# Attention scores from two query tiles stacked in the 128 rows, with the low part of k made after the transpose

## The chip, the cores and the metric

The kernel runs on one core of a Trainium2 chip. The metric is the device time of one execution in microseconds; the times below are medians of several executions of the same program. A profile is one further execution, recorded by the hardware profiler. Six actors matter: TensorE (PE, with its weight loads as PEld), VectorE (DVE), ScalarE (ACT), GpSimd (Pool), and the DMA queues, here issued by SyncE (SP). Each engine works through its own list of instructions in order, and semaphores tie the lists together.

## The reference

Three layers follow each other. The change touches the first alone: attention with normalised queries and keys, 4 x 12 = 48 heads of 448 tokens and 64 columns, in float32.

```python
def rmsnorm(x, g):
    rms = np.sqrt(np.mean(x * x, axis=-1, keepdims=True) + 1e-06)
    return x / rms * g
q_n, k_n = (rmsnorm(q, g_q), rmsnorm(k, g_k))
scores = (1.0 / np.sqrt(64)) * np.matmul(q_n, k_n.transpose(0, 1, 3, 2))
scores = scores - np.max(scores, axis=-1, keepdims=True)
attn = np.exp(scores)
attn = attn / (np.sum(attn, axis=-1, keepdims=True) + 1e-09)
out = np.matmul(attn, v)
```

Behind it come a mixture of 8 experts (each token goes to one) and a feed-forward layer of 768 x 2048. Both are left as they are.

## The kernel before

The kernel runs four stages in a row: `attention`, `routing`, `experts`, `feed_forward`. Attention loops over N = 48 heads. A head has T = 4 tiles of R = 112 tokens; D is 64. float32r matmuls take a float32 operand rounded to a shorter mantissa, so an operand is split into a high and a low part (`_hi`, `_lo`), whose products are summed in PSUM.

One head n goes through these steps; `m` is the loop variable, and each engine's loop (lines 197, 278, 363 and 458) sets its order by hand, with pieces of several heads in one iteration:

- ACT squares q and k (L311). DVE sums each row's 64 squares (L394). Pool turns the sums into 1/rms (L159, L161).
- Pool multiplies k by it (k_n, L177), again with a rounded output (the high half of `k_hl`, L183), and subtracts for the low half (L187). `k_hl` thus holds high and low side by side, 128 columns. Pool also writes the normalised q twice side by side into `q_n` (L193).
- PE transposes k's four tiles into the one bank `ps_tr` (L229); ACT copies them to `kT` (L329): rows 0 to 63 hold the high part, rows 64 to 127 the low part. Then PE transposes q's four tiles into the same bank (L236, it has to wait for `kT`); ACT rounds them to `qT_hi` and multiplies by the gain (L337); DVE makes `qT_lo` (L411).
- Scores: for each tile t one bank of `ps_s`, by two matmuls of 128 rows and 448 columns, `qT_hi` and `qT_lo` against `kT` (L221, L222).
- DVE takes the row maximum (L401), ACT the exponential with its row sum (L346), PE transposes it into `ps_pt` (L244, two banks in turn), ACT rounds (L355), DVE subtracts (L407). These four steps run once per tile.
- Values: eight matmuls of 112 rows and 448 columns into `ps_ux` (L258, L259), in two parts of four. ACT copies the result (`copy_u`, L317), PE multiplies by `mix` into the same bank (`outputs`, L266, eight instructions in the trace), and DVE scales it into `x_tok` (L421). v is split by ACT (L323, it waits for the values of the head before) and Pool (L147).

SP's queue loads q and k of head n once Pool has used those of head n-2, then v, then stores an older head. In one iteration, PE runs scores of tiles 2 and 3 (head m), the transposes of k (m+1), p of tile 0 (m), the first half of the values (m-1), the transposes of q (m+1), the second half of the values, p of tiles 1 and 2, scores of tiles 0 and 1 (m+1), p of tile 3 (m), and the outputs (m-1).

## Time and profile before

| what | value |
|---|---|
| median of 3 runs | 1293.96 us (1291.87 to 1294.43) |
| profiled execution, its own time | 1296.19 us |
| its span, first to last instruction | 1294.5 us |
| mean granted TensorE clock over the span | 0.973 |

The span lies 1.69 us under the profiled execution's own time, and that time 2.23 us over the median. Attention fills the span's first 350 us: the first exponential starts at 18.08 us, the last head's first one at 339.01 us. Rows of a timeline give start, duration, engine, line, operation and shapes. An engine's next instruction may start before the last has ended; so the cost of an instruction on its engine is the distance from its start to the next start, and its duration counts for whoever waits for the result. "Idle" in brackets is the engine's wait before the row, and who ended it.

### The profile page before, as it was taken

The page shows a single profiled execution, that of the slowest core. Times are in us where ns is not written, and L with a number is a line of the kernel's source. Part 1 is how long each engine was busy: PE and PEld are TensorE (multiplying, and loading weights), DVE is VectorE, ACT ScalarE, POOL GpSimd, SP SyncE. Part 2 cuts the span into 40 slices and gives each one's busy share as a digit, 9 for nine tenths or more (in the row PEclk, how much of TensorE's full clock was granted, in tenths as well). Part 3 has the DMA queues.
Part 4 walks back from the last instruction along what each step waited for, and adds up shares of the span by engine and source line. Part 5 has one row for each costly group of instructions (what it writes and reads, how often), then busy time and mean ns, then how long its engine had stood idle before and what let it go on. Part 6 is the DMA issues. An engine that isn't in the chain of part 4 may idle for free. (4 is left out here: it accounts for less than half of the span.)

```text
span 1294.5 us, 21003 instructions
## 1 busy us (share of the span) xinstructions
PE 1226.4 (95%) x6890; PEld 1097.1 (85%) x6890; DVE 894.2 (69%) x1257; ACT 757.6 (59%) x1434; POOL 553.3 (43%) x581
## 2 busy tenths in 40 slices
PE   5999999999748999999999995999999999999998
PEld 4888888888637988998899884999999999999997
DVE  4999999999757999999999973554432245552222
ACT  4999999999748777877787754222331122221111
POOL 6888888888335777667766740000000000000000
PEclk8999999999959999999999996999999999999999
DMA  1234333322103643664364014112232322211122
GB/s 50 75 103 116 97 105 93 83 67 72 29 28 120 244 142 128 244 244 147 124 242 147 38 49 122 49 49 62 74 92 62 91 65 74 70 44 49 56 86 73
DMA packets 99977, 126.42 MB, mean 98 GB/s; under 512 B 28568, under 2 KB 81048, under 8 KB 99872
## 3 DMA queue, kind: packets, MB, share of 16 engines
q1 hardware_dynamic: 92416, 103.07, 26.0%
q0 software_dynamic: 3360, 16.52, 3.5%
q10 hardware_dynamic: 4096, 5.51, 1.2%
q8 instruction: 57, 0.93, 0.3%
q14 instruction: 48, 0.39, 0.1%
HBM read 193.88 MB, written 19.27 MB: 165 GB/s over the span
## 5 line engine op out<-in xcount | busy, mean ns | idle before, releaser
L1010 ACT CAST w_hi<-w_raw 128x768 fp32r<-128x768 f32 (+1 forms) x294 | 249.7, 931 | 14.5 <-DMA w_raw<-moe_w_in 13.4
L1080 DVE TENSOR_TENSOR w_lo<-w_raw,w_hi 128x1024 fp32r<-128x1024 f32 x84 | 186.9, 2261 | 9.7 <-POOL w_lo L899 7.0
L1490 DVE TENSOR_TENSOR out_lo<-out_raw,out_hi 128x384 fp32r<-128x384 f32 x64 | 35.7, 558 | 169.5 <-ACT out_hi L1399 169.5
L1281 PE MATMUL ps_acc<-yT_hi,in_hi 128*128 128x448 f32 x384 | 142.9, 372 | 2.1 <-DVE yT_lo L1476 2.1
L899 POOL TENSOR_TENSOR w_lo<-w_raw,w_hi 128x1024 fp32r<-128x1024 f32 x42 | 105.8, 2520 | 91.3 <-ACT w_hi L1010 91.0
L1311 PE MATMUL ps_acc<-gT_hi,out_hi 128*128 128x448 f32 x384 | 142.6, 371 | 0.0
L1393 ACT ACTIVATE small_h<-ps_acc 128x448 f32<-128x448 f32 x64 | 34.9, 545 | 183.4 <-PE ps_acc L1283 183.4
L1282 PE MATMUL ps_acc<-yT_hi,in_lo 128*128 128x448 f32 x384 | 141.9, 370 | 0.0
L1283 PE MATMUL ps_acc<-yT_lo,in_hi 128*128 128x448 f32 x384 | 141.9, 369 | 0.0
L1313 PE MATMUL ps_acc<-gT_lo,out_hi 128*128 128x448 f32 x384 | 140.5, 366 | 0.0
L1312 PE MATMUL ps_acc<-gT_hi,out_lo 128*128 128x448 f32 x384 | 140.4, 366 | 0.0
L1399 ACT CAST out_hi<-out_raw 128x384 fp32r<-128x384 f32 x64 | 32.8, 513 | 179.9 <-PE ps_acc L1313 179.6
L1089 DVE TENSOR_TENSOR w_lo<-w_raw,w_hi 128x768 fp32r<-128x768 f32 x126 | 135.1, 1137 | 0.0
L407 DVE TENSOR_TENSOR pT_lo<-ps_pt,pT_hi 112x448 fp32r<-112x448 f32 x192 | 115.1, 620 | 27.6 <-ACT pT_hi L355 27.5
L346 ACT ACTIVATE probs<-ps_s,neg_max 112x448 f32<-112x448 f32 x192 | 122.7, 644 | 3.6 <-DVE neg_max L401 3.6
L1498 DVE TENSOR_TENSOR g_sb<-ps_acc,small_h 128x448 f32<-128x448 f32 x64 | 40.0, 625 | 116.3 <-ACT small_h L1393 116.3
L983 PE MATMUL ps_y<-w_hi,hT_hi 128*128 128x384 f32 x336 | 116.8, 348 | 1.5 <-issue 1.3
L893 POOL TENSOR_TENSOR w_lo<-w_raw,w_hi 128x768 fp32r<-128x768 f32 x42 | 105.7, 2518 | 22.9 <-ACT w_hi L1010 21.4
L401 DVE TENSOR_REDUCE neg_max<-ps_s 112x1 f32<-112x448 f32 x192 | 113.3, 610 | 2.0 <-PE ps_s L222 1.8
L984 PE MATMUL ps_y<-w_lo,hT_hi 128*128 128x384 f32 x336 | 113.5, 338 | 0.0
L985 PE MATMUL ps_y<-w_hi,hT_lo 128*128 128x384 f32 x336 | 113.5, 338 | 0.0
L953 PE MATMUL ps_h<-w_hi,xT_hi 128*128 128x512 f32 x252 | 101.3, 402 | 4.8 <-DVE w_lo L1080 2.9
(182 smaller groups left out, 2999.7 us busy)
## 6 DMA issues: line engine op xcount, KB each, us to landing
w_raw<-moe_w_in SPq DMA_DIRECT2D x84, 1536.0 KB
in_raw<-moe_w_in_in SPq DMA_DIRECT2D x32, 384.0 KB, 3.3
out_raw<-moe_w_out_in SPq DMA_DIRECT2D x64, 192.0 KB, 2.4
qk_raw<-q_in SPq DMA_DIRECT2D x48, 112.0 KB, 2.1
qk_raw<-k_in SPq DMA_DIRECT2D x48, 112.0 KB, 2.2
v_raw<-v_in SPq DMA_DIRECT2D x48, 112.0 KB, 2.0
x_rows<-x_tok SPq DMA_DIRECT2D x48, 112.0 KB, 2.5
out_rows<-o_sb ACTq DMA_DIRECT2D x26, 168.0 KB, 2.4
```

What stands on the lines that cost most here:

```text
L346: act.activation(probs[:, t, :], ps_s[0:R, t, 0:S], ACT.Exp, bias=neg_max[u][:, t:t + 1], accum_out=sums[u][:, t:t + 1]).then_inc(s_exp, 1)
L407: dve.tensor_tensor(pT_lo[u][:, :, cols], src, pT_hi[u][:, :, cols].bitcast(F32), ALU.subtract).then_inc(s_plo, 1)
L983: pe.matmul(out, hT_hi[u][:, c, :], w2_hi[:, c, cols], start=c == 0, stop=False)
L1010: act.copy(out[:, c, :], raw[:, c, :]).then_inc(s_hi, 1)
L1080: dve.tensor_tensor(w1_lo[:, c, :], w1_raw[:, c, :], w1_hi[:, c, :].bitcast(F32), ALU.subtract).then_inc(s_w1lo, 1)
L1089: dve.tensor_tensor(w2_lo[:, c, :], w2_raw[:, c, :], w2_hi[:, c, :].bitcast(F32), ALU.subtract).then_inc(s_w2lo, 1)
L1281: pe.matmul(h, in_hi[u][:, c, :], yT_hi[:, c, cols], start=c == 0, stop=False)
L1282: pe.matmul(h, in_lo[u][:, c, :], yT_hi[:, c, cols], start=False, stop=False)
L1283: last = pe.matmul(h, in_hi[u][:, c, :], yT_lo[:, c, cols], start=False, stop=c == C - 1)
L1311: pe.matmul(acc, out_hi[u][:, lhs], hi, start=first, stop=False)
L1312: pe.matmul(acc, out_lo[u][:, lhs], hi, start=False, stop=False)
L1313: last = pe.matmul(acc, out_hi[u][:, lhs], lo, start=False, stop=final)
```

## The change

Scores no longer contract 128 rows of high and low k. k is transposed unsplit, written twice side by side by Pool (`k_nn`), so that both halves of the 128 rows of the transposed bank hold the same 64 rows. ACT rounds this to `kT_hi`, and DVE subtracts to make `kT_lo` (new `split_k`, L411 of the kernel after; its instructions are 128x448). q is written once; one transpose takes two tiles of q side by side, so tile 2g lands in rows 0 to 63 and tile 2g+1 in rows 64 to 127, and `qT_hi`, `qT_lo` have 224 columns. For each pair g there are six matmuls of 64 rows and 448 columns, three into each of two banks, in turn from the upper and the lower rows. DVE's row sums of squares get their input halved by a new addition on Pool (`fold_squares`).

Orders change too: ACT's `square` stands at the end of the iteration, one head further ahead; PE's two halves of the values stand together ahead of the transposes of q; DVE's `split_k` stands behind the row maximum of tile 3.

```diff
@@ pool @@
+            def fold_squares(n, u):
+                pool.wait_ge(s_sq, n + 1)
+                if n > 1:
+                    pool.wait_ge(s_ss, n - 1)
+                pool.tensor_tensor(folded[u][:, :, :], squares[u][:, :, 0:D // 2], squares[u][:, :, D // 2:D], ALU.add).then_inc(s_fold, 1)
+
             def norm_k(n, u):
                 pool.wait_ge(s_r, n + 1)
-                if n > 0:
-                    pool.wait_ge(s_khl, n)
-                pool.tensor_tensor(k_n[:, :, :], qk_raw[u][:, 1, :, :], factors(u, 1), ALU.mult).then_inc(s_kn, 1)
-
-            def norm_k_hi(n, u):
-                pool.wait_ge(s_kn, n + 1)
                 if n > 1:
                     pool.wait_ge(s_trk, n - 1)
-                pool.tensor_tensor(k_hl[u][:, :, 0, :], qk_raw[u][:, 1, :, :], factors(u, 1), ALU.mult).then_inc(s_khi, 1)
-
-            def split_k(n, u):
-                pool.wait_ge(s_khi, n + 1)
-                pool.tensor_tensor(k_hl[u][:, :, 1, :], k_n[:, :, :], k_hl[u][:, :, 0, :].bitcast(F32), ALU.subtract).then_inc(s_khl, 1)
+                for a in range(2):
+                    last = pool.tensor_tensor(k_nn[u][:, :, a, :], qk_raw[u][:, 1, :, :], factors(u, 1), ALU.mult)
+                last.then_inc(s_kn, 1)
 
             def norm_q(n, u):
                 if n > 1:
                     pool.wait_ge(s_trq, n - 1)
-                for a in range(2):
-                    last = pool.tensor_tensor(q_n[u][:, :, a, :], qk_raw[u][:, 0, :, :], factors(u, 0), ALU.mult)
-                last.then_inc(s_qn, 1)
+                pool.tensor_tensor(q_n[u][:, :, :], qk_raw[u][:, 0, :, :], factors(u, 0), ALU.mult).then_inc(s_qn, 1)
...
@@ tensor @@
-            def scores(n, u, t):
+            def scores(n, u, g):
+
                 if n > 0:
-                    pe.wait_ge(s_exp, (n - 1) * T + t + 1)
-                if t == 0:
+                    pe.wait_ge(s_exp, (n - 1) * T + 2 * g + 2)
+                if g == 0:
                     pe.wait_ge(s_qlo, n + 1)
-                cols = slice(t * R, (t + 1) * R)
-                pe.matmul(ps_s[0:R, t, 0:S], qT_hi[u][:, cols], kT[u][:, :], start=True, stop=False)
-                pe.matmul(ps_s[0:R, t, 0:S], qT_lo[u][:, cols], kT[u][:, :], start=False, stop=True).then_inc(s_s, 1)
+                cols = slice(g * R, (g + 1) * R)
+                for i, (qT, kT) in enumerate(((qT_hi, kT_hi), (qT_hi, kT_lo), (qT_lo, kT_hi))):
+                    for half in range(2):
+                        rows = slice(half * D, (half + 1) * D)
+                        last = pe.matmul(ps_s[0:R, 2 * g + half, 0:S], qT[u][rows, cols], kT[u][rows, :], start=i == 0, stop=i == 2)
+                last.then_inc(s_s, 2)
...
             def transpose_q(n, u):
                 pe.wait_ge(s_qn, n + 1)
-                pe.wait_ge(s_kT, n + 1)
-                for t in range(T):
-                    last = pe.transpose(ps_tr[:, t * R:(t + 1) * R], q_n[u][:, t, :, :].rearrange("p a d -> p (a d)"), ident[0:R, 0:R])
+                pe.wait_ge(s_klo, n + 1)
+                for g in range(T // 2):
+                    two = q_n[u][:, 2 * g:2 * g + 2, :].rearrange("p a d -> p (a d)")
+                    last = pe.transpose(ps_tr[:, g * R:(g + 1) * R], two, ident[0:R, 0:R])
                 last.then_inc(s_trq, 1)
...
@@ scalar @@
-                act.copy(kT[u][:, :], ps_tr[:, 0:S]).then_inc(s_kT, 1)
+                act.copy(kT_hi[u][:, :], ps_tr[:, 0:S]).then_inc(s_khi, 1)
...
-                act.activation(qT_hi[u][:, :], ps_tr[:, 0:S], ACT.Copy, scale=gain[:, 0:1]).then_inc(s_qhi, 1)
+                act.activation(qT_hi[u][:, :], ps_tr[:, 0:S // 2], ACT.Copy, scale=gain[:, 0:1]).then_inc(s_qhi, 1)
...
@@ vector @@
-                dve.tensor_reduce(sumsq[u][:, :], squares[u][:, :, :], AX.X, ALU.add).then_inc(s_ss, 1)
+                dve.tensor_reduce(sumsq[u][:, :], folded[u][:, :, :], AX.X, ALU.add).then_inc(s_ss, 1)
...
+            def split_k(n, u):
+                dve.wait_ge(s_khi, n + 1)
+                dve.tensor_tensor(kT_lo[u][:, :], ps_tr[:, 0:S], kT_hi[u][:, :].bitcast(F32), ALU.subtract).then_inc(s_klo, 1)
```

**PE, middle of an iteration.** The rows stand from p of tile 0 to the end of the values; L244/L246 transpose p, L258 to L261 are the values, L236/L238 the transposes of q. Before:

```order
L244 MATMUL ps_pt<-ident,probs 112x112 x3
L258 MATMUL ps_ux<-pT_hi,v_hl 128x448 [waits s_vhl,s_plo,s_xc]
L259 MATMUL ps_ux<-pT_lo,v_hl 128x448
L258 MATMUL ps_ux<-pT_hi,v_hl 128x448
L259 MATMUL ps_ux<-pT_lo,v_hl 128x448
L236 MATMUL ps_tr<-ident,q_n 128x112 [waits s_kT,s_qn]
L236 MATMUL ps_tr<-ident,q_n 128x112 x3
L258 MATMUL ps_ux<-pT_hi,v_hl 128x448
L259 MATMUL ps_ux<-pT_lo,v_hl 128x448
L258 MATMUL ps_ux<-pT_hi,v_hl 128x448
L259 MATMUL ps_ux<-pT_lo,v_hl 128x448
```

After:

```order
L246 MATMUL ps_pt<-ident,probs 112x112 x3
L260 MATMUL ps_ux<-pT_hi,v_hl 128x448 [waits s_vhl,s_plo,s_xc]
L261 MATMUL ps_ux<-pT_lo,v_hl 128x448
L260 MATMUL ps_ux<-pT_hi,v_hl 128x448
L261 MATMUL ps_ux<-pT_lo,v_hl 128x448
L260 MATMUL ps_ux<-pT_hi,v_hl 128x448
L261 MATMUL ps_ux<-pT_lo,v_hl 128x448
L260 MATMUL ps_ux<-pT_hi,v_hl 128x448
L261 MATMUL ps_ux<-pT_lo,v_hl 128x448
L238 MATMUL ps_tr<-ident,q_n 128x112 [waits s_klo,s_qn]
L238 MATMUL ps_tr<-ident,q_n 128x112
```

The transposes of q have moved behind all eight matmuls of the values; they are two, not four, and wait for DVE's `s_klo` in place of ACT's `s_kT`.

**ACT, one iteration** from the exponential of tile 2 to the next copy of transposed k. L346/L345 are the exponentials, L355/L354 the rounding of p, L311/L310 the squares. Before:

```order
L346 ACTIVATE probs,sums<-ps_s,neg_max 112x448 [waits s_pt,s_max]
L355 CAST pT_hi<-ps_pt 112x4x112 [waits s_u,s_pt]
L337 ACTIVATE qT_hi<-ps_tr,gain 128x448 [waits s_s,s_trq]
L323 CAST v_hl<-v_raw 112x4x64 [waits s_u,s_v_in0]
L355 CAST pT_hi<-ps_pt 112x4x112 [waits s_pt]
L346 ACTIVATE probs,sums<-ps_s,neg_max 112x448 [waits s_pt,s_max]
L317 COPY u_sb<-ps_ux 128x448 [waits s_x,s_u]
L355 CAST pT_hi<-ps_pt 112x4x112 [waits s_pt] x2
L346 ACTIVATE probs,sums<-ps_s,neg_max 112x448 [waits s_se,s_pt,s_max]
L346 ACTIVATE probs,sums<-ps_s,neg_max 112x448 [waits s_pt,s_max]
L311 ACTIVATE squares<-qk_raw 112x512 [waits s_ss,s_qk_in0]
L329 CAST kT<-ps_tr 128x448 [waits s_s,s_trk]
```

After:

```order
L345 ACTIVATE probs,sums<-ps_s,neg_max 112x448 [waits s_pt,s_max]
L354 CAST pT_hi<-ps_pt 112x4x112 [waits s_u,s_pt]
L336 ACTIVATE qT_hi<-ps_tr,gain 128x224 [waits s_s,s_trq]
L322 CAST v_hl<-v_raw 112x4x64 [waits s_u,s_v_in0]
L354 CAST pT_hi<-ps_pt 112x4x112 [waits s_pt]
L310 ACTIVATE squares<-qk_raw 112x512 [waits s_fold,s_qk_in0]
L345 ACTIVATE probs,sums<-ps_s,neg_max 112x448 [waits s_pt,s_max]
L316 COPY u_sb<-ps_ux 128x448 [waits s_x,s_u]
L354 CAST pT_hi<-ps_pt 112x4x112 [waits s_pt] x2
L345 ACTIVATE probs,sums<-ps_s,neg_max 112x448 [waits s_se,s_pt,s_max]
L345 ACTIVATE probs,sums<-ps_s,neg_max 112x448 [waits s_pt,s_max]
L328 CAST kT_hi<-ps_tr 128x448 [waits s_s,s_trk]
```

The squares have moved from behind the exponential of tile 1 to a place between the copy of q and the exponential of tile 3.

**DVE, from the store of x to the split of q.** L401 is the row maximum, L407 the low part of p. Before:

```order
L421 TENSOR_TENSOR x_tok<-ps_ux,inv_sums 112x4x72 [waits s_rs,s_x]
L401 TENSOR_REDUCE neg_max<-ps_s 112x1 [waits s_s]
L394 TENSOR_REDUCE sumsq<-squares 112x8 [waits s_ms,s_sq]
L416 RECIPROCAL inv_sums<-sums_eps 112x4 [waits s_se]
L401 TENSOR_REDUCE neg_max<-ps_s 112x1 [waits s_s]
L407 TENSOR_TENSOR pT_lo<-ps_pt,pT_hi 112x4x112 [waits s_phi]
L411 SCALAR_TENSOR_TENSOR qT_lo<-ps_tr,gain,qT_hi 128x448 [waits s_qhi]
```

After:

```order
L425 TENSOR_TENSOR x_tok<-ps_ux,inv_sums 112x4x72 [waits s_rs,s_x]
L401 TENSOR_REDUCE neg_max<-ps_s 112x1 [waits s_s]
L394 TENSOR_REDUCE sumsq<-folded 112x8 [waits s_ms,s_fold]
L420 RECIPROCAL inv_sums<-sums_eps 112x4 [waits s_se]
L401 TENSOR_REDUCE neg_max<-ps_s 112x1 [waits s_s]
L411 TENSOR_TENSOR kT_lo<-ps_tr,kT_hi 128x448 [waits s_khi]
L407 TENSOR_TENSOR pT_lo<-ps_pt,pT_hi 112x4x112 [waits s_phi]
L415 SCALAR_TENSOR_TENSOR qT_lo<-ps_tr,gain,qT_hi 128x224 [waits s_qhi]
```

The new subtraction stands behind the row maximum of tile 3, ahead of the low part of p.

## Rows read from the trace of the kernel before

**Rows 1.** The page: span, then busy time of each engine.

```profile
span 1294.5 us, 21003 instructions
PE 1226.4 (95%) x6890; PEld 1097.1 (85%) x6890; DVE 894.2 (69%) x1257; ACT 757.6 (59%) x1434; POOL 553.3 (43%) x581
```

**Rows 2.** Busy time by stretch of attention; columns in the first row.

```profile
core 0: us, PE busy (x) PEld busy (x) DVE busy (x) ACT busy (x) POOL busy (x), PEclk, DMA share, GB/s
20.00:30.00 10.00, 8.22 (x44) 6.52 (x44) 8.03 (x14) 5.64 (x16) 5.92 (x10) 0.70 0.18 51
...
128.00:196.00 68.00, 67.73 (x485) 58.46 (x484) 61.87 (x122) 66.38 (x172) 57.78 (x92) 1.00 0.37 98
```

**Rows 3.** Line of the squares, 60 to 340 us: count, first and last start.

```profile
L311 ACT ACTIVATE squares<-qk_raw x40: 633/635/637, 64.2 to 326.8; 112x512 f32<-112x512 f32 x40
```

**Rows 4.** Timeline of PE, one head: start, us, engine, line, operation.

```profile
156.18 0.57 PE L244 MATMUL ps_pt<-ident,probs 112*112 112x112 f32 x4
156.59 0.92 PE L266 MATMUL ps_ux<-mix,u_sb 128*112 128x72 f32 x8
157.30 0.44 PE L221 MATMUL ps_s<-kT,qT_hi 128*112 128x448 f32 x1
...
158.20 0.55 PE L229 MATMUL ps_tr<-ident,k_hl 112*128 112x112 f32 x4
...
158.90 0.45 PE L258 MATMUL ps_ux<-pT_hi,v_hl 112*128 112x448 f32 x1
...
159.80 0.55 PE L236 MATMUL ps_tr<-ident,q_n 112*128 112x112 f32 x4
...
160.60 0.36 PE L258 MATMUL ps_ux<-pT_hi,v_hl 112*128 112x448 f32 x1
160.80 0.36 PE L259 MATMUL ps_ux<-pT_lo,v_hl 112*128 112x448 f32 x1
161.01 0.93 PE L244 MATMUL ps_pt<-ident,probs 112*112 112x112 f32 x8
```

**Rows 5.** Timeline of ACT, the same head.

```profile
155.27 0.64 ACT L346 ACTIVATE probs<-ps_s,neg_max 112x448 f32<-112x448 f32 x1
...
155.89 0.53 ACT L317 COPY u_sb<-ps_ux 128x448 f32<-128x448 f32 x1
160.41 0.68 ACT L337 ACTIVATE qT_hi<-ps_tr,gain 128x448 fp32r<-128x448 f32 x1
161.26 0.41 ACT L323 CAST v_hl<-v_raw 112x256 fp32r<-112x256 f32 x1 [0.17 <-PE ps_ux L259]
161.59 0.53 ACT L355 CAST pT_hi<-ps_pt 112x448 fp32r<-112x448 f32 x1
162.02 0.64 ACT L346 ACTIVATE probs<-ps_s,neg_max 112x448 f32<-112x448 f32 x1
```

**Rows 6.** Timeline of ACT in the last full head, which has no squares.

```profile
332.28 0.64 ACT L346 ACTIVATE probs<-ps_s,neg_max 112x448 f32<-112x448 f32 x1
...
333.84 0.53 ACT L329 CAST kT<-ps_tr 128x448 fp32r<-128x448 f32 x1 [0.21 <-PE ps_tr L229]
...
339.01 0.64 ACT L346 ACTIVATE probs<-ps_s,neg_max 112x448 f32<-112x448 f32 x1
```

**Rows 7.** Timeline of DVE, the head of rows 4.

```profile
157.01 1.15 DVE L407 TENSOR_TENSOR pT_lo<-ps_pt,pT_hi 112x448 fp32r<-112x448 f32 x2
...
158.44 0.61 DVE L401 TENSOR_REDUCE neg_max<-ps_s 112x1 f32<-112x448 f32 x1
159.11 0.69 DVE L394 TENSOR_REDUCE sumsq<-squares 112x8 f32<-112x512 f32 x1
...
159.80 0.60 DVE L401 TENSOR_REDUCE neg_max<-ps_s 112x1 f32<-112x448 f32 x1
```

**Rows 8.** SP's queue in the same head, then line L99's time from issue to landing.

```profile
159.37 0.43 SPq L99 DMA_DIRECT2D qk_raw<-k_in  x1
...
DMA to landing us min/median/max: 1.9/2.1/3.1
```

More of the change, by code:

```diff
@@ L46, in attention @@
         eps_d = sb("eps_d", [R, 2 * T])
-        q_n = [sb(f"q_n{u}", [R, T, 2, D]) for u in range(2)]
-        k_n = sb("k_n", [R, T, D])
-        k_hl = [sb(f"k_hl{u}", [R, T, 2, D], F32R) for u in range(2)]
+        folded = [sb(f"folded{u}", [R, 2 * T, D // 2]) for u in range(2)]
+        q_n = [sb(f"q_n{u}", [R, T, D]) for u in range(2)]
+        k_nn = [sb(f"k_nn{u}", [R, T, 2, D]) for u in range(2)]
         v_hl = [sb(f"v_hl{u}", [R, T, 2, D], F32R) for u in range(2)]
-        kT = [sb(f"kT{u}", [P, S], F32R) for u in range(2)]
-        qT_hi = [sb(f"qT_hi{u}", [P, S], F32R) for u in range(2)]
-        qT_lo = [sb(f"qT_lo{u}", [P, S], F32R) for u in range(2)]
+        kT_hi = [sb(f"kT_hi{u}", [P, S], F32R) for u in range(2)]
+        kT_lo = [sb(f"kT_lo{u}", [P, S], F32R) for u in range(2)]
+        qT_hi = [sb(f"qT_hi{u}", [P, S // 2], F32R) for u in range(2)]
+        qT_lo = [sb(f"qT_lo{u}", [P, S // 2], F32R) for u in range(2)]
         neg_max = [sb(f"neg_max{u}", [R, T]) for u in range(2)]
@@ L80, in attention @@
         s_v_in = [sem(f"s_v_in{u}") for u in range(2)]
[L81 to L83 removed]
+        s_half, s_sq, s_fold, s_ss, s_ms, s_r = (sem(x) for x in ("s_half", "s_sq", "s_fold", "s_ss", "s_ms", "s_r"))
+        s_qn, s_kn, s_vhi, s_vhl = (sem(x) for x in ("s_qn", "s_kn", "s_vhi", "s_vhl"))
+        s_trk, s_khi, s_klo, s_trq, s_qhi, s_qlo = (sem(x) for x in ("s_trk", "s_khi", "s_klo", "s_trq", "s_qhi", "s_qlo"))
         s_s, s_max, s_exp, s_pt, s_phi, s_plo = (sem(x) for x in ("s_s", "s_max", "s_exp", "s_pt", "s_phi", "s_plo"))
@@ L191, in norm_q @@
                     pool.wait_ge(s_trq, n - 1)
-                for a in range(2):
-                    last = pool.tensor_tensor(q_n[u][:, :, a, :], qk_raw[u][:, 0, :, :], factors(u, 0), ALU.mult)
-                last.then_inc(s_qn, 1)
+                pool.tensor_tensor(q_n[u][:, :, :], qk_raw[u][:, 0, :, :], factors(u, 0), ALU.mult).then_inc(s_qn, 1)
             pool.wait_ge(s_half, 3)
             for m in range(-2, N):
+                if m + 2 < N:
+                    fold_squares(m + 2, (m + 2) % 2)
                 if 0 <= m + 1 < N:
-                    split_k(m + 1, (m + 1) % 2)
                     norm_q(m + 1, (m + 1) % 2)
@@ L228, in transpose_k @@
                 for t in range(T):
-                    last = pe.transpose(ps_tr[:, t * R:(t + 1) * R], k_hl[u][:, t, :, :].bitcast(F32).rearrange("p a d -> p (a d)"), ident[0:R, 0:R])
+                    last = pe.transpose(ps_tr[:, t * R:(t + 1) * R], k_nn[u][:, t, :, :].rearrange("p a d -> p (a d)"), ident[0:R, 0:R])
                 last.then_inc(s_trk, 1)
@@ L279, in _ @@
                 if 0 <= m < N:
-                    scores(m, m % 2, 2)
-                    scores(m, m % 2, 3)
+                    scores(m, m % 2, 1)
                 if m + 1 < N:
@@ L287, in _ @@
                     values(m - 1, (m - 1) % 2, 0)
+                    values(m - 1, (m - 1) % 2, 1)
                 if m + 1 < N:
                     transpose_q(m + 1, (m + 1) % 2)
-                if m - 1 >= 0:
-                    values(m - 1, (m - 1) % 2, 1)
                 if 0 <= m < N:
@@ L296, in _ @@
                     scores(m + 1, (m + 1) % 2, 0)
-                    scores(m + 1, (m + 1) % 2, 1)
                 if 0 <= m < N:
@@ L386, in _ @@
                     split_hi(m, m % 2, 1)
+                if m + 3 < N:
+                    square(m + 3, (m + 3) % 2)
+                    square_emb(m + 3, (m + 3) % 2)
         @block.vector
@@ L472, in _ @@
                     row_max(m, m % 2, 3)
+                if 0 <= m + 1 < N:
+                    split_k(m + 1, (m + 1) % 2)
+                if 0 <= m < N:
                     split_lo(m, m % 2, 0)
```

16 lines of the change are left out of this document (5 added, 11 removed).

## The prediction

> **What bounds the kernel now.** The page comes first: PE 95%, DVE 69%, ACT 59% of the span [rows 1]. That is an average over four stages, and only attention is touched, so the busy time by stretch comes next. In attention, PE, ACT and DVE are all nearly full: of 68 us, PE 67.7, ACT 66.4, DVE 61.9, Pool 57.8, at a granted clock of 1.00 [rows 2]. Such a row doesn't say who is the bound, because a matmul's duration overlaps the next one's. The squares, one per head, recur 39 times from 64.2 to 326.8 us: 6.73 us a head [rows 3]. The question is what sets that 6.73.
>
> The timeline answers it. Rows 4 (PE) and 5 (ACT) close a loop, each step starting as its predecessor releases it:
> - ACT starts the exponential of tile 3 at 155.27; PE transposes it at 156.18 (0.91).
> - PE in order: outputs 156.59, scores of tiles 2 and 3 157.30, transposes of k 158.20, p of tile 0, values 158.90, transposes of q 159.80, then the second half of the values with its last matmul at 160.80. From 156.18 that is 4.62.
> - ACT's copy of v waits for that last matmul (the row shows the wait) and starts at 161.26 (0.46); rounding 161.59; next exponential of tile 3 162.02 (0.76).
>
> 0.91 + 4.62 + 0.46 + 0.76 = 6.75. **The bound is this loop through PE and ACT**, no engine alone. The last full head confirms it: it has no squares, so ACT has some 0.5 us less to do, yet its period is 339.01 - 332.28 = 6.73; ACT merely waits for PE ahead of the copy of k [rows 6]. Work taken from ACT or Pool buys nothing here unless it stands in the loop. So each part of the change is asked: which loop does it enter or leave?
>
> **The change, part by part.**
>
> *Values ahead of the transposes of q (PE).* Before, four matmuls stood between p of tile 0 and the transposes of q; after, eight. Four take 158.90 to 159.80, 0.90; eight in one run have one fewer change of kind, so 0.90 + 4 x 0.20 (160.60 to 160.80) = 1.70 to 1.80 with the four taken at 0.90 again. I take 1.74 [rows 4]. The values don't leave the loop; but the copy of q, which was beside it, now comes into it: ACT can't reach the copy of v until it has copied q, and q's transposes now come last on PE.
>
> *Transposes of q.* From start to ACT's copy it is 159.80 to 160.41, 0.61 [rows 4, 5]. Two fewer instructions: four take 0.55 and eight 0.93, so 0.095 each, 0.19 less. 0.42; ACT's own order may have held the copy, so 0.40.
>
> *Copy of q, 224 columns instead of 448.* ACT's copies take 0.41 us at 256 columns and 0.53 at 448 [rows 5], 0.625 ns a column: 0.68 falls by 0.14 to 0.54. The next one starts some 0.1 before the end (161.59 + 0.53 against 162.02): 0.42 or so.
>
> *Squares moved.* They stood on ACT at a place where it could afford them; now they stand between the copy of q and the exponential of tile 3, inside the loop. A plain copy of 448 columns holds ACT 0.43 (161.59 to 162.02), and 64 more columns at 0.625 ns make it 0.47; with the activation's longer fixed part I take 0.52. Their load is needed earlier. Key loads are issued at 159.37 and land 1.9 to 3.1 later [rows 8], by 162.5; the squares would come about 1 us after the copy of q, at about 162.6 on the same clock once that copy is as late as worked out here. Just covered at the longest landing, free at the median; without cover it would add what is missing, some tenths.
>
> *Scores.* Now 157.30 to 158.20, 0.90 for four matmuls [rows 4]; after, six of 64 rows in three pairs. No row shows two matmuls side by side. If a pair costs one matmul (0.205): 0.90 - 0.205 = 0.69. If the six run one after the other: 0.90 + 2 x 0.205 = 1.31. I take 0.25 a pair, near the low end, since the two use different rows and banks but each needs its own weight load: 0.82. The TensorE page of the Trainium skill ("TensorE: Matmul & The Clock Gate", Part 3, packing small matmuls) says that matmuls in different row groups do run together, which is the low end, 0.69.
>
> *The sum for this loop*, exponential of tile 3 to the next: 0.91, then PE from 156.18 to 157.30 1.12, scores 0.82, transposes of k and p 158.20 to 158.90 0.70, values 1.74, to the copy of q 0.40, copy 0.42, copy of v 0.33 (161.26 to 161.59), rounding 0.43, squares 0.52. That is **7.39** (7.26 with pairs at 0.205).
>
> *split_k on DVE opens a second loop.* It starts when the row maximum of tile 3 is done. Before, that maximum starts 2.79 after the first low part of p (157.01 to 159.80) [rows 7]. DVE no longer waits for the squares (158.44 + 0.53 = 158.97, not 159.11: 0.14) and sums half as many: 0.69 for 512 columns against 0.61 for 448 is 1.25 ns a column, and the distance of 0.53 for 448 allows 1.18 at most; some of it is fixed, so I take 1.05 for each of 256 columns, 0.27 less. 2.79 - 0.14 - 0.27 = 2.38. Then the maximum 0.53 and split_k 0.62 (1.15 for two low parts of p less their distance of 0.53; the same 448 columns) [rows 7]. A hand-over from DVE to PE isn't in the rows; the one from PE to ACT is 0.10 (160.80 + 0.36 to 161.26), so 0.12. Then 0.40 to the copy of q, 0.42 + 0.33 + 0.43 + 0.52 to the exponential as above, 0.62 for that (155.27 to 155.89) and 0.42 for the copy behind it, 0.57 from a rounding of p to its low part (0.53 and a hand-over, estimated) [rows 5]. Sum **7.36**. So both loops meet near 7.4, and shortening either alone gives little.
>
> *Pool.* It loses a subtraction of k and a multiplication of q and gains one addition, so it is less full than the 57.8 of 68 us of rows 2, and it stands in neither loop. The squares that the addition waits for are made a head earlier, and that head's time hides it; without this it would stand with its some 0.6 in the second loop. I take nothing.
>
> *Sum.* 7.39 - 6.75 = 0.64 us a head. The regular stretch is from about 40 us to 339 us, 45 heads: **+29 us**. The first heads, with the array partly at the lower clock [rows 2], lose one step (k's subtraction on Pool) and gain another (split_k): nothing either way, 2 us for the range. Against the profiled execution, 1296.19 + 29 = 1325.5; against the median, 1293.96 + 29 = 1323.
>
> **Rivals.**
>
> *A. The score blocks cost more.* With matmuls of a pair one after another the first loop is 7.39 + 0.49 = 7.88, or +1.13 x 45 = 51: 1345. A change from 128-row to 64-row use may also cost something; a matmul lasts 0.36 and hands over after 0.20, so waiting for an empty array is 0.16, twice in the loop: 7.71, +43: 1337. For it: six instructions and six weight loads in place of four. Against: separate rows and banks. "TensorEngine Tiling (Array Packing)" of the Trainium skill, Key Properties, does state that a change of tiling mode drains the array, which would make this rival's 1337 the outcome; no run here shows one, and the gaps of rows 4 at changes of kind (0.90 for four matmuls, not 0.82) show a smaller price.
>
> *B. Faster: ACT becomes the bound.* Should the two loops not bind, because the queues run far enough apart for PE to be ahead, ACT's own work would rule: 6.75 less the 0.17 wait [rows 5], less 0.14 in the copy of q, 6.44; -0.31 x 45 = -14: 1280. The point from which it decides is where q's transposes start: no later than 2.5 us after the scores of tile 2, as before (157.30 to 159.80) [rows 4]. Rows 6 speak against it: less ACT work gave no time. And PE has 4.4 us of work in the first loop, all of it in order behind the exponential of tile 3.
>
> *C. The moves cancel*: both loops at 6.70 to 6.80, within 2.6 us of before: 1294. It needs 0.6 us of error in sums whose steps are nearly all rows.
>
> *D. The clock.* PE has more gaps; in the first stretch a granted clock of 0.70 goes with PE busy 8.2 of 10 us [rows 2]. PE would be idle some 1.4 of 7.4 us, spread in pieces under 1 us. If attention ran at the lower level, the PE part of the loop (4.4) would grow by well over half: 1400 and more.
>
> **Numbers.** Forecast 0.62; A 0.20; B 0.08; C 0.03; D and other large losses 0.07. The likeliest case gives 1323 us. The range goes from 1308 (pairs at 0.205, and the copy of q, the way to it and the squares each 0.1 shorter, which leaves the second loop at 7.06, +14) to 1347 (A without any pairing, and 2 for the first heads), and leaves out B, C and D. A measurement of this kernel can tell about 0.2% (2.6 us) from no change. Slower 0.89 (forecast, A, D), same 0.03 (C), faster 0.08 (B).
>
> **What the profile after would show.** The squares recur every 7.4 us, not 6.73. ACT waits close to 1 us a head ahead of the copy of q, put down to PE's transposes; DVE waits ahead of the split of q; PE waits ahead of the transposes of q (for DVE's new subtraction) or not at all, and ahead of p of tile 3. A score block takes 0.8 us on PE (0.7: pairs free; 1.3: no pairing). If the copy of q has no wait and the period is under 6.75, the loops were misread. If ACT waits ahead of the squares for a DMA, the load's cover was too thin.

## The result and the profile after

The changed kernel takes **1325.83 us** (median of 4 runs, 1325.58 to 1330.17), before 1294.20 us (1291.87 to 1297.30): a ratio of 1.0251, interval 1.0221 to 1.0281. It is 32 us slower. The forecast was 1323 us, range 1308 to 1347.

The page after, its span, busy times and clock row:

```profile
span 1324.1 us, 21194 instructions
PE 1222.3 (92%) x6986; PEld 1077.5 (81%) x6986; DVE 903.3 (68%) x1305; ACT 751.2 (57%) x1434; POOL 525.6 (40%) x533
PEclk8999999999966999999999997999999999999999
```

Against [rows 1], PE, ACT and Pool have less busy time (DVE has 9 us more, for the new subtraction), and the span is 29.6 us longer. Most of the work went down and the waits went up. Busy time by stretch, the same 68 us as in [rows 2] (the same columns):

```profile
128.00:196.00 68.00, 60.77 (x463) 49.48 (x463) 58.15 (x120) 59.28 (x157) 47.30 (x74) 1.00 0.34 93
```

The line of the squares, as in [rows 3]:

```profile
L310 ACT ACTIVATE squares<-qk_raw x37: 632/642/647, 62.8 to 328.6; 112x512 f32<-112x512 f32 x37
```

PE has 60.8 of 68 us where it had 67.7, at the same granted clock of 1.00. The squares recur every (328.6 - 62.8) / 36 = **7.38 us**; before, every 6.73. 0.65 x 45 heads is 29 us, nearly the whole difference of the spans. Attention's last instruction, DVE's scaling into `x_tok`, ends at 350.3 us before and 380.6 after; the stages behind it take 944.1 and 943.4.

PE's timeline after, one head (the piece that answers [rows 4]):

```profile
167.55 0.60 PE L246 MATMUL ps_pt<-ident,probs 112*112 112x112 f32 x4 [0.43 <-ACT probs L345]
167.98 0.99 PE L268 MATMUL ps_ux<-mix,u_sb 128*112 128x72 f32 x8
168.90 0.46 PE L222 MATMUL ps_s<-kT_hi,qT_hi 64*112 64x448 f32 x2
169.20 0.37 PE L222 MATMUL ps_s<-kT_lo,qT_hi 64*112 64x448 f32 x2
169.40 0.37 PE L222 MATMUL ps_s<-kT_hi,qT_lo 64*112 64x448 f32 x2
169.70 0.60 PE L230 MATMUL ps_tr<-ident,k_nn 112*128 112x112 f32 x4
...
170.46 0.45 PE L260 MATMUL ps_ux<-pT_hi,v_hl 112*128 112x448 f32 x1
...
171.97 0.36 PE L261 MATMUL ps_ux<-pT_lo,v_hl 112*128 112x448 f32 x1
172.18 0.35 PE L238 MATMUL ps_tr<-ident,q_n 112*128 112x112 f32 x2
```

ACT's timeline after (answers [rows 5]), and DVE's split_k:

```profile
166.77 0.63 ACT L345 ACTIVATE probs<-ps_s,neg_max 112x448 f32<-112x448 f32 x1
...
167.38 0.54 ACT L316 COPY u_sb<-ps_ux 128x448 f32<-128x448 f32 x1
...
172.57 0.45 ACT L336 ACTIVATE qT_hi<-ps_tr,gain 128x224 fp32r<-128x224 f32 x1 [0.64 <-PE ps_tr L238]
172.91 0.40 ACT L322 CAST v_hl<-v_raw 112x256 fp32r<-112x256 f32 x1
173.21 0.54 ACT L354 CAST pT_hi<-ps_pt 112x448 fp32r<-112x448 f32 x1
173.63 0.64 ACT L310 ACTIVATE squares<-qk_raw 112x512 f32<-112x512 f32 x1
174.17 0.63 ACT L345 ACTIVATE probs<-ps_s,neg_max 112x448 f32<-112x448 f32 x1
```

```profile
171.27 0.61 DVE L411 TENSOR_TENSOR kT_lo<-ps_tr,kT_hi 128x448 fp32r<-128x448 f32 x1
```

The loop can be read off: exponential of tile 3 166.77, its transposes on PE ("p of tile 3") 167.55, outputs, scores, transposes of k 169.70, values 170.46, q's transposes 172.18, copy of q 172.57, copy of v, rounding, squares, exponential 174.17. That is 7.40 us, and each step starts on an earlier one of the loop or, at the outputs, on the copy of u, which stands right behind the same exponential. ACT waits 0.64 ahead of the copy of q and 0.31 ahead of the copy of k, where the prediction had put close to 1 us on the first alone. split_k ends at 171.88, 0.3 ahead of q's transposes, which start 0.21 behind PE's last matmul: a hand-over from DVE to PE takes 0.15 (split of q, 173.05 + 0.45, to the scores at 173.65), so the first loop decides and the second, through DVE, is some 0.15 us behind.

### The profile page after: what moved, and what is told of

The parts are those of the page before. It is cut to its first block and busy times, and to the rows that moved or that the text cites. A ratio compares the mean times of both kernels' runs of the same rounds, so it can differ in the third digit from the quotient of the medians.

```text
span 1324.1 us, 21194 instructions
## 1 busy us (share of the span) xinstructions
PE 1222.3 (92%) x6986; PEld 1077.5 (81%) x6986; DVE 903.3 (68%) x1305; ACT 751.2 (57%) x1434; POOL 525.6 (40%) x533
## 5 line engine op out<-in xcount | busy, mean ns | idle before, releaser
L407 DVE TENSOR_TENSOR pT_lo<-ps_pt,pT_hi 112x448 fp32r<-112x448 f32 x192 | 115.5, 622 | 22.3 <-ACT pT_hi L354 16.0
L345 ACT ACTIVATE probs<-ps_s,neg_max 112x448 f32<-112x448 f32 x192 | 123.4, 657 | 3.5 <-DVE neg_max L401 3.5
L401 DVE TENSOR_REDUCE neg_max<-ps_s 112x1 f32<-112x448 f32 x192 | 113.6, 613 | 9.3 <-PE ps_s L222 4.5
L246 PE MATMUL ps_pt<-ident,probs 112*112 112x112 f32 x768 | 101.3, 265 | 20.0 <-ACT probs L345 19.2
```

The costliest lines, as they stand in the source:

```text
L345: act.activation(probs[:, t, :], ps_s[0:R, t, 0:S], ACT.Exp, bias=neg_max[u][:, t:t + 1], accum_out=sums[u][:, t:t + 1]).then_inc(s_exp, 1)
L407: dve.tensor_tensor(pT_lo[u][:, :, cols], src, pT_hi[u][:, :, cols].bitcast(F32), ALU.subtract).then_inc(s_plo, 1)
```

## Experiments

The question has two parts: do the moved steps cost what the loops say, and what are the new ingredients (64-row matmuls, split_k, the addition on Pool) worth by themselves? (split_k and the narrower copy of q have no run of their own.) The period is read from the line of the squares in each run's trace, as above.

### One step at a time, on the kernel before

**The squares alone moved to the end of ACT's iteration**, one head further ahead:

```diff
+            square(0, 0)
             for m in range(-2, N + 2):
...
-                if m + 2 < N:
-                    square(m + 2, (m + 2) % 2)
-                    square_emb(m + 2, (m + 2) % 2)
...
                     split_hi(m, m % 2, 1)
+                if m + 3 < N:
+                    square(m + 3, (m + 3) % 2)
+                    square_emb(m + 3, (m + 3) % 2)
```

> The kernel before with one step of the change alone: ACT's squares moved to the end of the iteration, one head further ahead. Theory (the squares enter the loop that sets the period): +0.5 us a head, 7.25 instead of 6.75, +22 to +24 us: about 1317. Rival (ACT has spare time before, so 0.5 us of its work can stand anywhere): no change, 1294.

Measured 1318.81 us, ratio 1.0191 (1.0171 to 1.0210). The line of the squares:

```profile
L311 ACT ACTIVATE squares<-qk_raw x38: 630/636/638, 60.4 to 328.6; 112x512 f32<-112x512 f32 x38
```

268.2 / 37 = 7.25 us a head, as expected. In its timeline, ACT's exponential of tile 3 and copy of u, then PE's transposes of p behind it, outputs and scores:

```profile
170.01 0.63 ACT L346 ACTIVATE probs<-ps_s,neg_max 112x448 f32<-112x448 f32 x1
...
170.62 0.53 ACT L317 COPY u_sb<-ps_ux 128x448 f32<-128x448 f32 x1
```

```profile
170.78 0.59 PE L244 MATMUL ps_pt<-ident,probs 112*112 112x112 f32 x4 [0.40 <-ACT probs L346]
171.21 1.00 PE L266 MATMUL ps_ux<-mix,u_sb 128*112 128x72 f32 x8
172.01 0.44 PE L221 MATMUL ps_s<-kT,qT_hi 128*112 128x448 f32 x1
```

The same instructions, one of them 3 us later in the list, cost 0.5 us a head. The outputs now start 0.06 behind the end of the copy of u (170.62 + 0.53), and it takes 0.80 from them to the scores where it took 0.71 [rows 4]: later on ACT also means later there. ACT's spare time (the copy of k waits 0.2 in this run) is of no use to a step that stands in the loop.

**q's transposes alone moved behind the values**:

```diff
                     values(m - 1, (m - 1) % 2, 0)
+                    values(m - 1, (m - 1) % 2, 1)
                 if m + 1 < N:
                     transpose_q(m + 1, (m + 1) % 2)
-                if m - 1 >= 0:
-                    values(m - 1, (m - 1) % 2, 1)
```

> The kernel before with one step of the change alone: PE's transposes of q behind all eight matmuls of the values. Theory (the copy of q enters the loop): the PE part from p of tile 3 to q's transposes 4.4 to 4.5 us, then 0.58, 0.56, 0.33 and 1.33 to the next p of tile 3: 7.2 to 7.5 us a head, +22 to +34 us, 1316 to 1328. Rival (PE has the same work as before, only in another order): 1294.

Measured 1325.47 us, ratio 1.0236 (1.0210 to 1.0263); the squares recur 36 times from 64.6 to 329.8, 7.37 us a head. ACT waits 0.65 ahead of the copy of q, and the scores of tiles 0 and 1 behind it wait 0.77 for the split of q (ACT's timeline, then PE's from the head before):

```profile
170.50 0.63 ACT L336 ACTIVATE qT_hi<-ps_tr,gain 128x448 fp32r<-128x448 f32 x1 [0.65 <-PE ps_tr L236]
```

```profile
164.63 0.43 PE L221 MATMUL ps_s<-kT,qT_hi 128*112 128x448 f32 x1 [0.75 <-DVE qT_lo L410]
...
165.51 0.55 PE L244 MATMUL ps_pt<-ident,probs 112*112 112x112 f32 x4
...
169.92 0.55 PE L236 MATMUL ps_tr<-ident,q_n 112*128 112x112 f32 x4
...
172.00 0.43 PE L221 MATMUL ps_s<-kT,qT_hi 128*112 128x448 f32 x1 [0.77 <-DVE qT_lo L410]
```

The cost is the expected one, the way to it is not. p of tile 3 (165.51) waits for nothing here, so the exponential doesn't stand in the loop that decides. That loop is a third one: q's transposes 169.92, copy of q 170.50, split of q on DVE, scores 172.00, then PE without a stop to the next transposes of q (164.63 to 169.92): 0.58 + 1.50 + 5.29 = 7.37. After the whole change it isn't the one that decides: copy and split of q have half the columns there, and PE waits 0.43 ahead of p of tile 3.

Each of the two moves alone thus costs nearly as much as the whole change (25 and 31 us of 32). They don't add up: they lengthen different loops, the squares that of the exponential, q's transposes most of all that of q's split, in which the squares don't stand. And the rest of the change takes time out again, 0.20 in the copy of q (0.54 to the next start, then 0.34) and 0.19 from the start of q's transposes to that copy (0.58, then 0.39). The score blocks give nothing back: from the outputs to the transposes of k it is 1.61 before (156.59 to 158.20) and 1.72 after (167.98 to 169.70).

### One step back, on the kernel after

**Squares back, out of the loop.** On ACT ahead of the exponential of tile 0 and of their own head; DVE's sum behind split_k, so that it doesn't wait for Pool:

```diff
-            square(0, 0)
...
+                if m + 2 < N:
+                    square(m + 2, (m + 2) % 2)
+                    square_emb(m + 2, (m + 2) % 2)
                 if 0 <= m < N:
                     exp(m, m % 2, 0)
...
-                if m + 3 < N:
-                    square(m + 3, (m + 3) % 2)
-                    square_emb(m + 3, (m + 3) % 2)
...
-                if m + 2 < N:
-                    sum_squares(m + 2, (m + 2) % 2)
-                    prepare(m + 2, (m + 2) % 2)
...
                     split_k(m + 1, (m + 1) % 2)
+                if m + 2 < N:
+                    sum_squares(m + 2, (m + 2) % 2)
+                    prepare(m + 2, (m + 2) % 2)
```

> The changed kernel with the squares back to their own head and ahead of the exponential of tile 0 on ACT, out of both loops, and DVE's sum of squares moved behind split_k so that it need not wait for Pool's addition. Theory: 0.4 to 0.5 us a head less, about 6.95, -18 to -20 us: about 1307. Still over before, since values, split_k and the mode changes stay. Rival (the squares are not in the loop): 1326.

Measured 1303.84 us, ratio 1.0063 (1.0044 to 1.0082); 38 periods from 64.0 to 325.7, 6.89 us a head. Some two thirds of the loss are gone. The run undoes two things, and no run parts them; by the sums it is the squares: the first loop without their 0.54 is 6.85, while the second had 0.15 to spare even before its sum was moved. So with the other steps in place, the squares' place was worth 22 us.

**q's transposes back between the halves of the values**, the move of the second diff undone:

> The changed kernel with q's transposes put back between the two halves of the values on PE. Theory (two loops meet at 7.4 us a head; split_k on DVE is the later one): PE now reaches q's transposes 0.8 us sooner but must wait there until split_k is done, and the second half of the values stands behind that wait, so the copy of v and all behind it come later. 7.9 us a head instead of 7.39, +25 us: about 1350. Rival (the four matmuls moved ahead of q's transposes are themselves the cost): a head falls by 0.8 us, to 6.6, and the time to about 1290.

Measured 1345.62 us, ratio 1.0396 (1.0377 to 1.0415), 33 periods from 65.1 to 324.1, 7.85 us a head. PE's row says why:

```profile
172.92 0.38 PE L238 MATMUL ps_tr<-ident,q_n 112*128 112x112 f32 x2 [0.52 <-DVE kT_lo L412]
```

PE stands 0.5 us until split_k is done, with half of the values behind it, and the copy of v behind those. The move that costs 31 us in the kernel before saves 20 here: splitting k on DVE makes q's transposes late, and the place of the transposes had to follow.

**Without Pool's addition**; DVE sums all 64 squares:

```diff
-                if m + 2 < N:
-                    fold_squares(m + 2, (m + 2) % 2)
...
-                dve.wait_ge(s_fold, n + 1)
+                dve.wait_ge(s_sq, n + 1)
...
-                dve.tensor_reduce(sumsq[u][:, :], folded[u][:, :, :], AX.X, ALU.add).then_inc(s_ss, 1)
+                dve.tensor_reduce(sumsq[u][:, :], squares[u][:, :, :], AX.X, ALU.add).then_inc(s_ss, 1)
```

> The changed kernel without Pool's addition: DVE sums all 64 squares of a row again. Theory (the sum stands in the second loop, through split_k): that loop grows by 0.27 us from 7.25 to about 7.5, so +0.13 to +0.17 us a head, +6 to +8 us: about 1333. Rival (the sum's input size is off the path): 1326.

Measured 1331.13 us, ratio 1.0272 (1.0246 to 1.0299); 35 periods from 63.4 to 327.7, 7.55 us a head, 0.17 more. The second loop, through DVE, now decides, and it was 0.10 to 0.15 below the first. (The medians differ by 5 us, attention's ends in the two traces by 7.5: the stages behind it differ by some us from run to run, 941 to 948 in all of these traces.)

### What the 64-row matmuls cost

**Pairs apart.** Three matmuls into one bank first, then the three into the other:

```diff
-                for i, (qT, kT) in enumerate(((qT_hi, kT_hi), (qT_hi, kT_lo), (qT_lo, kT_hi))):
-                    for half in range(2):
+                for half in range(2):
+                    for i, (qT, kT) in enumerate(((qT_hi, kT_hi), (qT_hi, kT_lo), (qT_lo, kT_hi))):
```

> The changed kernel with the six matmuls of a score block in another order: three into one bank, then three into the other, so that no two neighbours use different rows. Theory (neighbours in different rows run side by side, a pair at the price of one): the block grows by 3 x 0.2 = 0.6 us, in the loop once and beside it once; 8.0 to 8.15 us a head, +28 to +36 us: about 1357. Rival (the array runs them one by one anyway, or in any order): no change, 1326.

Measured 1326.54 us, ratio 1.0239 (1.0218 to 1.0259), 7.39 us a head. **The expectation fell, and the rival held.** The trace, sorted by start, reads as that of the kernel after:

```profile
170.01 0.46 PE L222 MATMUL ps_s<-kT_hi,qT_hi 64*112 64x448 f32 x2
170.31 0.37 PE L222 MATMUL ps_s<-kT_lo,qT_hi 64*112 64x448 f32 x2
170.51 0.37 PE L222 MATMUL ps_s<-kT_hi,qT_lo 64*112 64x448 f32 x2
170.81 0.60 PE L230 MATMUL ps_tr<-ident,k_nn 112*128 112x112 f32 x4
```

In the program the first matmul of the second bank stands behind all three of the first; in the trace each kind of matmul starts twice at once, so the second bank's first starts beside the first bank's first. (Starts are measured; the ends of matmuls are modelled, so the trace tells nothing of their order.) So the question was open again: are the rows what lets two run together, or is a 64-row matmul cheap in itself?

**All on the same rows** (it leaves out the scores of every second tile, which get their neighbour's):

```diff
-                        rows = slice(half * D, (half + 1) * D)
+                        rows = slice(0, D)
```

> The changed kernel with all six matmuls of a block reading rows 0 to 63 (tiles 2g+1 get the scores of tile 2g: only the time is read). Theory (different rows are what lets two matmuls run side by side; the order in the program does not matter, as the run with the pairs apart showed): they run one by one, 1.3 us a block instead of 0.7, 8.0 to 8.15 us a head, +28 to +36 us: about 1357. Rival (64-row matmuls are cheap in themselves, or the banks decide): 1326.

Measured 1358.72 us, ratio 1.0494 (1.0472 to 1.0515), 33 periods from 62.1 to 326.0, 8.00 us a head:

```profile
168.72 0.65 PE L222 MATMUL ps_s<-kT_hi,qT_hi 64*112 64x448 f32 x2
169.21 0.58 PE L222 MATMUL ps_s<-kT_lo,qT_hi 64*112 64x448 f32 x2
169.63 0.56 PE L222 MATMUL ps_s<-kT_hi,qT_lo 64*112 64x448 f32 x2
170.12 0.60 PE L230 MATMUL ps_tr<-ident,k_nn 112*128 112x112 f32 x4
```

The block takes 1.40 us in place of 0.80, 0.42 a pair in place of 0.20. The banks and the number of matmuls are the same, so the rows decide. Stacking two tiles saves 33 us against 64-row matmuls that don't pair; without it the loss would be some 65, not 32.

**No change between 128 and 64 rows** (it leaves out half of the matmuls and adds up the products of two tiles):

```diff
-                    for half in range(2):
-                        rows = slice(half * D, (half + 1) * D)
-                        last = pe.matmul(ps_s[0:R, 2 * g + half, 0:S], qT[u][rows, cols], kT[u][rows, :], start=i == 0, stop=i == 2)
+                    last = pe.matmul(ps_s[0:R, 2 * g + i % 2, 0:S], qT[u][:, cols], kT[u][:, :], start=i < 2, stop=i > 0)
```

> The changed kernel with each pair of 64-row matmuls replaced by one of all 128 rows, into the same two banks: the scores are not what they should be (two tiles' products are summed, and three matmuls stand for six), only the time is read. The count of slots in PE's queue that a pair takes, 0.2 us, stays, and no change between 128 and 64 rows is left. Theory (a change of rows empties the array, 0.1 to 0.2 us each): from the outputs' start to the transposes of k 1.40 us instead of 1.72; the second loop, 7.25, then decides, so 7.2 to 7.3 us a head, -4 to -8 us: about 1320. Rival (the longer gaps belong to the matmuls themselves): 1326.

Measured 1318.41 us, ratio 1.0179 (1.0161 to 1.0197), 36 periods from 62.8 to 325.2, 7.29 us a head:

```profile
166.87 1.00 PE L266 MATMUL ps_ux<-mix,u_sb 128*112 128x72 f32 x8
167.67 0.44 PE L220 MATMUL ps_s<-kT_hi,qT_hi 128*112 128x448 f32 x1
...
168.35 0.55 PE L228 MATMUL ps_tr<-ident,k_nn 112*128 112x112 f32 x4
...
170.57 0.37 PE L259 MATMUL ps_ux<-pT_lo,v_hl 112*128 112x448 f32 x1
170.92 0.38 PE L236 MATMUL ps_tr<-ident,q_n 112*128 112x112 f32 x2
```

From outputs to scores 0.80 (after: 0.92), from scores to the transposes of k 0.68 (after: 0.80): **0.12 us for each change of rows, 0.24 a block**, of the 0.32 expected. The other 0.09 from outputs to scores, against 0.71 of [rows 4], isn't due to the rows: it goes with the copy of u. In this run, in the kernel after (167.38 + 0.54, outputs 167.98) and in the run with the squares moved alone, the outputs start 0.06 behind that copy's end; where it ends earlier, in the kernel before and with q's transposes moved alone, the distance is 0.71 to 0.72. So a score block saves one slot of 0.20 and pays 0.24 for its two changes. The loop gives back only 0.09 of the 0.24, since q's transposes now start 0.35 behind the last matmul in place of 0.21: they wait for split_k. The second loop decides, at 7.29. (0.09 x 45 is 4 us; the medians differ by 7.)

### The same work in another order

If places and not work made the loss, the changed kernel's instructions should do better in another order. All functions are those of the change; only the lists differ (entries are function, head, tile or part):

```python
# PE
(transpose_k, m + 1, ()), (before_p, m, (0,)), (before_p, m, (1,)), (values, m - 1, (0,)),
(transpose_q, m + 1, ()), (values, m - 1, (1,)), (before_p, m, (2,)), (scores, m + 1, (0,)),
(before_p, m, (3,)), (scores, m + 1, (1,)), (outputs, m - 1, ())
# ACT
(split_hi, m - 1, (3,)), (squares_of, m + 2, ()), (exp, m, (0,)), (exp, m, (1,)),
(copy_k, m + 1, ()), (split_hi, m, (0,)), (exp, m, (2,)), (copy_q, m + 1, ()),
(split_hi, m, (1,)), (exp, m, (3,)), (split_v, m + 1, ()), (copy_u, m - 1, ()),
(split_hi, m, (2,))
# DVE
(maximum, m, (1,)), (low_p, m - 1, (2,)), (maximum, m, (2,)), (low_p, m - 1, (3,)),
(store_x, m - 2, ()), (sums_of, m + 2, ()), (split_k, m + 1, ()), (low_p, m, (0,)),
(invert_sums, m - 1, ()), (maximum, m, (3,)), (split_q, m + 1, ()), (low_p, m, (1,)),
(maximum, m + 1, (0,))
```

(`before_p` is `transpose_p`, `low_p` is `split_lo`, `maximum` is `row_max`, `squares_of` and `sums_of` are `square` and `sum_squares`, each with its part of the setup.)

> The changed kernel's instructions, all of them, in another order: on PE both score blocks of a head stand behind p of tiles 2 and 3, ahead of the outputs, and q's transposes between the halves of the values; on ACT the squares stand ahead of the exponential of tile 0; on DVE split_k stands ahead of the row maximum of tile 3. Theory (the change lost by the places of its steps in the two loops, not by its amount of work): 6.6 us a head instead of 7.39, -35 us against the changed kernel, 1291, about 3 under before. Rival (the new work itself, split_k and the mode changes, costs more than it saves whatever the order): not under 1300.

Measured **1285.02 us**, ratio 0.9927 (0.9909 to 0.9944): 11 us under the kernel before, which took 1296.01 beside it, and 41 under the change. 39 periods from 60.8 to 316.6, 6.56 us a head. ACT's waits there:

```profile
169.31 0.45 ACT L326 ACTIVATE qT_hi<-ps_tr,gain 128x224 fp32r<-128x224 f32 x1 [0.23 <-PE ps_tr L238]
169.65 0.52 ACT L344 CAST pT_hi<-ps_pt 112x448 fp32r<-112x448 f32 x1
170.06 0.65 ACT L335 ACTIVATE probs<-ps_s,neg_max 112x448 f32<-112x448 f32 x1
...
170.69 0.41 ACT L312 CAST v_hl<-v_raw 112x256 fp32r<-112x256 f32 x1
```

One short wait for q's transposes is left, and neither copy of v nor squares stand between the copy of q and the exponential of tile 3. A further order, with that exponential and the roundings further from what they wait for (PE's list as above):

```python
# ACT
(split_hi, m - 1, (3,)), (exp, m, (0,)), (exp, m, (1,)), (copy_k, m + 1, ()), (exp, m, (2,)),
(split_hi, m, (0,)), (split_hi, m, (1,)), (copy_q, m + 1, ()), (exp, m, (3,)),
(split_v, m + 1, ()), (split_hi, m, (2,)), (copy_u, m - 1, ()), (squares_of, m + 3, ())
# DVE
(low_p, m - 1, (0,)), (split_q, m, ()), (invert_sums, m - 2, ()), (low_p, m - 1, (1,)),
(low_p, m - 1, (2,)), (maximum, m, (0,)), (maximum, m, (1,)), (low_p, m - 1, (3,)),
(maximum, m, (2,)), (store_x, m - 2, ()), (sums_of, m + 2, ()), (split_k, m + 1, ()),
(maximum, m, (3,))
```

> As the run before, with the exponential of tile 3 and the rounding of tiles 1 and 2 further apart from what they wait for, squares at the end of ACT's iteration, and the row maximum of tile 3 at the end of DVE's. Theory: 6.5 us a head, 1285, about 9 under before: the loops are then near ACT's own work of about 6.4. Rival as before: not under 1300.

Measured 1285.03 us, ratio 0.9921 (0.9902 to 0.9939), 39 periods from 60.1 to 315.5, 6.55 us a head. The time is the expected 1285, the further gain over the first order isn't there. ACT's copies and exponentials last up to 0.58 and 0.70 us in it (0.54 and 0.64 in the kernel after), but the next instruction starts 0.42 and 0.52 behind them as ever, so that isn't the reason. PE is. In the first order it is busy in all 68.00 of the 68 us of [rows 2] and its queue shows no wait between 60 and 320 us. Two of its rows there:

```profile
167.20 1.04 PE L246 MATMUL ps_pt<-ident,probs 112*112 112x112 f32 x8
168.01 0.46 PE L260 MATMUL ps_ux<-pT_hi,v_hl 112*128 112x448 f32 x1
```

The eight transposes of p take 0.81 to the next start, in the further order 0.70 (167.32 to 168.02): some 0.1 is the only stop in the head, p of tile 1 waiting for DVE's low part of p of tile 3 (166.89 + 0.61, and 0.15 for the hand-over). The further order has a stop of 0.1 too, ahead of the scores of tiles 0 and 1 (0.58 from p of tile 2, 163.39 to 163.97, against 0.48, 163.37 to 163.85). So PE's own list, by its spacing, takes some 6.45 us (an estimate: 6.56 less the stop), and no order of this list could win more than 0.1 us a head, 5 us.

**The old instructions in such an order** (both pairs of score tiles behind p of tiles 2 and 3, ahead of the outputs; k's transposes right behind the outputs; squares ahead of the exponential of tile 0; every function that of the kernel before):

> The kernel before, its instructions unchanged, in an order like that of the reordered kernel that ran at 1285: both score blocks behind p of tiles 2 and 3 and ahead of the outputs, squares ahead of the exponential of tile 0. Theory (the change's ingredients are worth something once they stand well: a shorter copy and split of q, two transposes and a fourth of the score slots less): the old instructions gain little from the order, 6.65 to 6.75 us a head, 1290 to 1295. Rival (only the order paid, the ingredients nothing): about 1285 here too.

Measured 1298.92 us, ratio 1.0036 (1.0022 to 1.0049), 39 periods from 61.4 to 329.8, 6.88 us a head: worse than expected, and no gain. The waits show what stands in the way, the sum over 39 heads (0.27 a head):

```profile
PEld ps_tr L229 <- POOL k_hl L187: 10.7, 39, 0.3
```

k's transposes stand earlier in this order and meet Pool's subtraction of k, which the change has taken off Pool. So this order doesn't make the gain alone, nor do the ingredients alone. (The two orders aren't the same in each place, so how much of 1298.9 against 1285.0 is which ingredient's stays open; and whether some other order of the old instructions would reach 1285 was not tried.)

**The good order without Pool's addition** (the diff of the run without it above, on this kernel):

> The reordered kernel that ran at 1285 without Pool's addition. Theory (the sum still stands ahead of split_k on DVE): +0.2 us a head, +9 us: about 1294. Rival (DVE waits 0.5 us a head for the scores there, which covers 0.27): 1285.

Measured 1297.02 us, ratio 1.0015 (1.0002 to 1.0028), 39 periods from 64.1 to 329.9, 6.82 us a head, 0.26 more than with it. DVE's rows:

```profile
165.35 1.16 DVE L376 TENSOR_REDUCE neg_max<-ps_s 112x1 f32<-112x448 f32 x2 [0.49 <-PE ps_s L220]
...
168.38 0.68 DVE L369 TENSOR_REDUCE sumsq<-squares 112x8 f32<-112x512 f32 x1
168.97 0.61 DVE L386 TENSOR_TENSOR kT_lo<-ps_tr,kT_hi 128x448 fp32r<-128x448 f32 x1
```

DVE's wait of 0.49 isn't a cover: it stands behind split_k in the loop and stays 0.49 (0.48 with the addition). 0.26 of the 0.27 of the longer sum comes through. The loop through PE and DVE had next to nothing to spare here. So in this order the addition on Pool is worth 12 us (14 against the kernels before that ran beside each); in the order of the change it was worth 5 to 8.

## Why the prediction was right

**The bound.** Loop and period held: 6.73 before, and after the change each step of the predicted loop stands in the trace. The squares moved alone changed the period as that loop demands; q's transposes moved alone cost what was expected, but through the split of q and the scores, a third loop that the prediction didn't have. One link was misread. From the exponential of tile 3 to p's transposes the prediction took 0.91 as ACT's. After, and in the run with the squares moved alone, that link is 0.78 and 0.77: 166.77 to 167.55, 170.01 to 170.78. In the kernel before, PE was waiting for DVE's low part of p of tile 1 there, which ends at 156.03, 0.15 ahead of it:

```profile
155.41 0.62 DVE L407 TENSOR_TENSOR pT_lo<-ps_pt,pT_hi 112x448 fp32r<-112x448 f32 x1 [0.36 <-ACT pT_hi L355]
```

Both ways start at the rounding of p of tile 1, so the sum of before closed at 6.75 in spite of it.

**The first loop, term by term** (expected, then after): exponential to p 0.91, 0.78; p to the outputs to the scores 1.12, 1.35; score block 0.82, 0.80; transposes of k and p 0.70, 0.76; values 1.74, 1.72; to the copy of q 0.40, 0.39; copy 0.42, 0.34; copy of v 0.33, 0.30; rounding 0.43, 0.42; squares 0.52, 0.54. Sum 7.39, 7.40. That it came out to 0.01 is luck in part: 0.30 too much in seven terms, most of it the misread link (0.13) and the copy of q (0.08), against 0.31 too little in three, nearly all of it at the changes between outputs, scores and transposes (0.23 and 0.06). The prediction priced those changes at nothing in its sum, and left out that the outputs also wait for the copy of u.

**The score block.** 0.25 a pair was a guess near the low end of 0.205 to 0.41; it is 0.20, the lower bound (the change of rows behind it fills the block to 0.80). The rival of 64-row matmuls that don't pair, priced at 7.88 and 1345, came true only where it was forced: 8.00 and 1358.72, with a block of 1.40 where 1.31 was priced. The other half of that rival, a price for each change of rows, is real with 0.12 where 0.16 was the estimate, twice in the loop; that the time didn't go to its 1337 is due to the free pairs and to the terms that were too long. "TensorEngine Tiling (Array Packing)" of the Trainium skill, Key Properties, states that a change of tiling mode drains the array, without a price. These runs agree that the change costs time; a drain as such no trace shows.

**The second loop.** 7.36 expected; the run without a change of rows shows 7.29. It is close behind the first, as said: removing 0.24 from the first loop gave 0.09, and adding 0.27 to the second cost 0.17. The copy of q (0.34, not 0.42) is most of the 0.07.

**Squares and their load.** The term was right, 0.54, and the load was covered: between 60 and 330 us the changed kernel shows no wait of ACT for a DMA there, and the worst other run, the further order, two of 1.2 us together. **Pool**: as said, in neither loop. But "nothing" was too short for its addition: it takes 0.27 out of DVE's part of the second loop, worth 5 to 8 us. The prediction had this saving in the sum of the second loop, not under Pool.

**Rivals.** Faster with ACT as the bound: 6.44 a head was out of reach in this order, as the rows of the last full head said, and 6.55 is what a better order reaches, with PE's own list as the bound and not ACT's; the rival hadn't counted PE's. The granted clock stayed at 1.00 in the stretch of [rows 2] with PE busy 60.8 of 68 us.

**The size.** 0.64 x 45 = 29 was forecast, the spans differ by 29.6 and the medians by 31.6.

## What to carry to other kernels

When several engines are all over 90% busy, write down the loop: start to start, across engines, from one instruction to its next instance, until the steps add up to the period. A step costs its length if it stands in that loop and nothing if it doesn't, whatever its engine's spare time; so a change with less work but two steps moved into the loop was 32 us slower, and the same instructions in another order were 11 us faster than before. Price a change of place as carefully as a change of work, and look for the second loop before you count on removing the first; a third may hold when you move one step alone. When one engine's instructions follow each other without a stop, as PE's in the good order, reordering has nothing left to give.
